# Bias features on three engines, with a second table of logarithms in PSUM, and half of the early weight loads issued later

## The chip, the cores and the metric

The kernel runs on one core of a Trainium2 chip. A core has five engines that work side by side, each through its own list of instructions, in order: TensorE (matrix products, PE in the rows; PEld is its loading of weights), VectorE (DVE), ScalarE (ACT), GpSimd (POOL) and SyncE (SP), which here issues all transfers. Engines meet only through semaphores: an instruction waits until a counter has reached a value, and raises another when it is done. SBUF is the on-chip memory that all of them use; PSUM is the memory that TensorE writes its results to, eight banks of 512 float32 columns on each of 128 partitions, which VectorE and ScalarE also read and write. The metric is device time in microseconds (us) of one execution; lower is better.

## The reference, cut to what matters

Attention with a learned bias on the distance of two positions, followed by two dense layers. What the change touches is the bias:

```python
rel = pos[:, None] - pos[None, :]                  # 576 x 576
psi_rel = log1p(abs(rel))
psi_i = log1p(maximum(pos[:, None], 1.0))
x = (psi_rel / psi_i)[..., None]
h = maximum(x @ w1 + b1, 0.0)                      # 32 hidden units
bias = h @ w2                                      # one number for each of 8 heads
scores = scale * q @ k.T + bias
attn = softmax(scores); out = attn @ v             # 4 sequences, 8 heads, 64 wide
x = (g := x @ w_in) - tanh(g);  x = x @ w_out      # first dense layer
x = (silu(x @ w_gate) * (x @ w_val)) @ w_out2      # second dense layer
```

The bias doesn't depend on the sequence. It is made once, written to memory, and read back for each tile of scores.

## The kernel before, in words

The kernel has three stages. The bias stage takes the first 70 us; then come the attention of the first eight heads without any dense work beside it (to about 130 us), attention and the first dense layer interleaved, and the second dense layer.

**The bias stage.** The logarithm of |row - column| depends on the difference alone, so one table of logarithms (`table`, 1080 columns, each partition with its own shift) holds all rows: a row's logarithms are 576 neighbouring columns of it. Each partition stands for one hidden unit of one of four rows, so that one instruction over 128 x 576 makes 32 hidden units for four rows: a *feature*, max(table x scale, -b1) on VectorE or relu(table x scale + b1) on ScalarE, where scale holds w1 divided by the row's own logarithm. Scale and b1 are operands of one column, [P,1]. VectorE's form lacks the term + b1, which is added as a constant (`fold`) when the result is evacuated.

A *round* is four features, 16 rows. There are 36 rounds (`NQUAD`); six rounds (`GQ`) are one block of 96 rows. In each round:

- VectorE makes features 0 to 2 (`features`, L1073), ScalarE feature 3 (L765), into one of two buffers, `feat[:, par]`, with par the round's parity. Both wait until TensorE has finished round r-2, which read the same buffer (semaphore `e_feat`).
- TensorE (L1345 to L1355) waits for the features and for the evacuation of round r-2, multiplies by w2 in eight matmuls into one of two pairs of PSUM banks, `ps_s` and `ps_y[:, 0:2]`.
- ScalarE evacuates the round before (`evacuate`, L753) into one of six buffers, behind its own feature of this round.
- Every second round SP stores two rounds to memory in four DMAs (`store_bias`, L480); behind rounds 1, 3, 5, 9, 13, 17, 21 and 25 it issues a load of one 512 KB chunk of the first dense layer's weights (`load_w1`, L476). Behind round 27 it issues the first loads of the attention stage (`load_bias`, `load_k`, `load_q`).

The table is made in two parts: the columns that the first six rounds read first, and the rest (0 to `LATE`) during round 0. Rounds from `GQ` on wait for both (`act_tab`, `dve_rest`).

Some small pieces of later work are put into these lists by hand: ScalarE's `q_high` behind its part of rounds 8 and 18 and VectorE's `q_low` (L1082) one round later, ScalarE's `w1_high` in rounds 20 to 23 and VectorE's `w1_low` (L1068) in rounds 21 to 24. `q_low` and `w1_low` read two tensors from SBUF. GpSimd splits two k matrices into a high and a low part at the start (`split_k`, L651) and then has nothing to do until the attention's first `norm` (L671).

**Weights.** The first dense layer's 16 chunks go to a buffer of their own each. Eight are loaded in the bias stage and eight in the interleaved stage, two behind the loads of each head from the tenth on (L587). `w1_high` and `w1_low` split them, 4 tiles in the bias stage and 4 in each interleaved slot, so that one slot uses up two chunks.

**The order** on each engine is written out by hand in these loops; nothing is planned at run time.

Of the kernel before, what the change touches and what calls it, by code (L numbers as in the profile page):

```python
# [27 lines left out]
B, H, S, D = 4, 8, 576, 64  # L28
# [20 lines left out]
GQ = 6  # L49
# [76 lines left out]
def attention_layers_kernel(nc, q_t, k_t, v_p, rowc, w1c, b1c, w2sel, w1_chunks, w2_chunks, out, bias_d, y_d):  # L126
    ctx = ExitStack()
    with ctx:
# [3 lines left out]
        def sem(name):  # L132
            return ctx.enter_context(nc.semaphore(name))
# [20 lines left out]
        with nc.sbuf_tensor("feat", [P, 2, 4, S], F32) as feat:  # L154
# [62 lines left out]
        ps_pt = ctx.enter_context(nc.psum_tensor("ps_pt", [P, 512], F32))  # L217
        ps_s = ctx.enter_context(nc.psum_tensor("ps_s", [P, 2, 512], F32))
        bias_ps = [ps_s, ps_y[:, 0:2, :]]
        gate_ps = [ps_h[:, 0:T2], ps_s[:, 0, 0:T2]]  # L220
        val_ps = [ps_pt[:, 0:T2], ps_s[:, 1, 0:T2]]

# [4 lines left out]
        d_bias = [sem(f"d_bias{i}") for i in range(BR)]  # L227
        d_bias_out, d_y_first, d_y_rest, d_y_in, d_out = [sem(f"d_bias_out{i}") for i in range(EV)], sem("d_y_first"), sem("d_y_rest"), sem("d_y_in"), sem("d_out")
        pool_tab, dve_tab, dve_rest, dve_b, act_tab = (sem(x) for x in ("pool_tab", "dve_tab", "dve_rest", "dve_b", "act_tab"))
        a_feat, v_feat, e_feat, a_bias, e_fold, v_fold = (sem(x) for x in (  # L230
            "a_feat", "v_feat", "e_feat", "a_bias", "e_fold", "v_fold"))
        a_w1hi, v_w1lo, p_w1lo = sem("a_w1hi"), sem("v_w1lo"), sem("p_w1lo")
        a_w2hi, v_w2lo = sem("a_w2hi"), sem("v_w2lo")
        e_score, v_score, a_exp, v_den, v_inv, p_norm = (sem(x) for x in (
# [26 lines left out]
        def bias_groups(rnd):  # L261

            tile, qi = divmod(rnd, GQ)
            return [(tile * ROWSTEP + qi + gg * GQ, TABC - tile * QT - qi - gg * GQ) for gg in range(4)]

        V_FEAT, A_FEAT = (3, 3), (1, 1)

        def feat_done(rnd, per):

            return sum(per[r % 2] for r in range(rnd + 1))  # L270

        def w1_at(k):

# [5 lines left out]

        Q_AT = (8, 18)  # L280
        W1_FIRST, W1_PART, W1_AT = 4, 4, 20
        W1_EARLY, W1_LOAD_AT = 8, (1, 3, 5, 9, 13, 17, 21, 25)
        BIAS_LOADS = 27

        def w1_tiles(moe):
# [184 lines left out]
        def _(eng):  # L470
# [99 lines left out]
            for n in range(H, NH):  # L570
                hd = HEADS[n]
                if hd.unit > 1 and n == FIRST_OF[hd.unit] + 1:
                    store_y(hd.unit - 2, 0)
                load_v(hd)
                following = HEADS[n + 2:n + 3]
                for nxt in following:
                    if not ended(hd):
                        load_q(nxt)
                for t in range(hd.nt):
                    load_bias(hd.tile0 + t + BR)  # L580
                    if t == 1 and hd.unit > 1 and n == FIRST_OF[hd.unit] + 1:
                        store_y(hd.unit - 2, 1)
                for nxt in following:
                    load_k(nxt)
                    if ended(hd):
                        load_q(nxt)
                for c in islice(w1_left, 2 if n > H else 0):  # L587
                    load_w1(c)


# [46 lines left out]
        def _(eng):  # L637
# [84 lines left out]

            split_k(HEADS[0], [])
            split_k(HEADS[1], [])
            eng.wait_ge(e_feat, NQUAD)
            eng.sem_inc(p_glo, CR)
            eng.sem_inc(p_alo, 1)
# [12 lines left out]
        def _(eng):  # L740
# [12 lines left out]
            def evacuate(rnd):  # L753
                par = rnd % 2
                eng.wait_ge(e_feat, rnd + 1)
                if rnd >= 2 * EV and par == 0:
                    eng.wait_ge(d_bias_out[rnd // 2 % EV], 64 * (rnd // 2 // EV))
                eng.activation(pairs(bias_ev[rnd // 2 % EV][:, par, :]), bias_ps[par][:, :, 0:T1], ACT.Identity,
                               bias=fold[:, par:par + 1]).then_inc(a_bias, 1)

            def w1_high(k):
                eng.wait_ge(d_w1[k // 4], 32)
# [2 lines left out]
            def features(rnd):  # L765
                par = rnd % 2
                if rnd >= 2:
                    eng.wait_ge(e_feat, rnd - 1)
                for gg in range(V_FEAT[par], 4):
                    g, col = bias_groups(rnd)[gg]  # L770
                    eng.activation(feat[:, par, gg, :], table[:, col:col + S], ACT.Relu,
                                   scale=scale_t[:, g:g + 1], bias=b1_col).then_inc(a_feat, 1)
# [5 lines left out]
            eng.wait_ge(dve_rest, 2)  # L778
            eng.activation(table[:, 0:LATE], table2[:, 0:LATE], ACT.Ln, bias=1.0).then_inc(act_tab, 1)
            eng.wait_ge(v_fold, 1)  # L780
            for rnd in range(1, NQUAD):
                if rnd == GQ:
                    eng.wait_ge(act_tab, 3)
                    eng.wait_ge(dve_rest, 4)
                features(rnd)
                evacuate(rnd - 1)
                if W1_AT <= rnd < W1_AT + W1_FIRST:
                    w1_high(rnd - W1_AT)
                if rnd in Q_AT:
                    q_high(HEADS[Q_AT.index(rnd)], [])  # L790
# [240 lines left out]
        def _(eng):  # L1031
# [25 lines left out]
            def fold_terms():  # L1057

                eng.tensor_copy(b_cols[:, 0:1], b1_col).then_inc(dve_b, 1)
                eng.tensor_copy(b_cols[:, 1:2], b1_col).then_inc(dve_b, 1)  # L1060
                eng.memset(b_cols[:, 2:4], 0.0).then_inc(dve_b, 1)
                eng.wait_ge(pool_tab, 3)
                distances(slice(0, LATE), dve_rest, 0)
                scales(REST, dve_rest, 2)
                eng.wait_ge(e_fold, 1)
                eng.tensor_copy(fold[:, :], ps_h[:, 0:2]).then_inc(v_fold, 1)
# [6 lines left out]
            def features(rnd):  # L1073
                par = rnd % 2
                if rnd >= 2:
                    eng.wait_ge(e_feat, rnd - 1)
                for gg in range(V_FEAT[par]):
                    g, col = bias_groups(rnd)[gg]
                    eng.tensor_scalar(feat[:, par, gg, :], table[:, col:col + S], scale_t[:, g:g + 1],  # L1079
                                      neg_b1, ALU.mult, ALU.max).then_inc(v_feat, 1)  # L1080

            def q_low(hd, moe):  # L1082
# [7 lines left out]
            eng.wait_ge(dve_tab, 6)  # L1090
            for rnd in range(NQUAD):
                if rnd == GQ:
                    eng.wait_ge(act_tab, 3)
                    eng.wait_ge(dve_rest, 4)
                features(rnd)
                if rnd == 0:
                    fold_terms()
                if W1_AT < rnd <= W1_AT + W1_FIRST:
                    w1_low(rnd - W1_AT - 1)
                if rnd - 1 in Q_AT:  # L1100
                    q_low(HEADS[Q_AT.index(rnd - 1)], [])
# [233 lines left out]
        def _(eng):  # L1335
# [2 lines left out]
            eng.wait_ge(pool_tab, 5)  # L1338

            for gg in range(4):  # L1340
                at = max(0, gg - 1)
                mm = eng.matmul(ps_h[32 * gg:32 * gg + 32, 0:2], sel, b_cols[:, at:at + 2], start=True, stop=True)
            mm.then_inc(e_fold, 1)

            for rnd in range(NQUAD):  # L1345
                par = rnd % 2
                if rnd >= 2:
                    eng.wait_ge(a_bias, rnd - 1)
                eng.wait_ge(v_feat, feat_done(rnd, V_FEAT))
                eng.wait_ge(a_feat, feat_done(rnd, A_FEAT))  # L1350
                for a in range(2):
                    for gg in range(4):
                        mm = eng.matmul(bias_ps[par][32 * gg:32 * gg + 32, a, 0:T1], sel,
                                        feat[:, par, gg, a * T1:(a + 1) * T1], start=True, stop=True)
                mm.then_inc(e_feat, 1)  # L1355
# [283 lines left out]
```

## Time and profile before

| | |
|---|---|
| time, median of 3 runs | 1228.98 us (1228.85 to 1229.46) |
| the profiled execution's own time | 1227.36 us |
| its span, first to last instruction | 1225.5 us |
| busy: TensorE, VectorE, ScalarE, GpSimd | 1176.1, 605.9, 573.2, 525.3 us |
| granted TensorE clock | full speed throughout |
| DMA | 125.46 MB, 102 GB/s on average |

The profile is one execution, recorded by the hardware. An instruction's row gives its start and its duration; the durations of neighbours on an engine overlap a little, so the distance from one start to the next is what an instruction costs in a row of its kind. "[1.46 <-PE ...]" behind a row says how long the engine stood idle ahead of it and which engine ended the wait. The chain of waits starts at the last instruction and goes back, at each step, to what released it. A piece of that chain is work that nothing hid. Rows of one line and kind that follow each other are merged, with their count (x30).

### The profile page before, as it was taken

How to read it: one execution, taken by the hardware profiler on the slowest of the kernel's cores; microseconds unless marked ns; L12 is line 12 of the kernel's file. 1: busy time of each engine (PE TensorE's matmuls, PEld its weight loads, DVE VectorE, ACT ScalarE, POOL GpSimd, SP SyncE). 2: the span in 40 equal slices, each digit the busy share in tenths (PEclk: the TensorE clock that was granted, in tenths of full speed). 3: DMA queues.
4: the chain of work that ended last, by engine and by line, in shares of the span. 5: the costliest groups of instructions: out<-in, count | busy, mean ns of one | idle time of the engine just before them, and what ended most of it. 6: DMA issues, size and time to landing. Idle time of an engine off the chain costs nothing.

```text
span 1225.5 us, 20261 instructions
## 1 busy us (share of the span) xinstructions
PE 1176.1 (96%) x7320; PEld 1079.1 (88%) x7320; DVE 605.9 (49%) x1377; ACT 573.2 (47%) x1163; POOL 525.3 (43%) x584
## 2 busy tenths in 40 slices
PE   5778899999999999999999999999999999999998
PEld 2345699999999998999899999999999999999998
DVE  8967777766665666666666534321211212122111
ACT  6977677665565555555555554422212222121212
POOL 2036577765565557777777622111111111111111
PEclk9999999999999999999999999999999999999999
DMA  5888565353444335455555344200000000000000
GB/s 182 262 253 236 151 197 151 111 146 109 121 134 122 108 89 149 134 140 138 149 140 139 117 143 141 66 26 27 27 1 26 27 26 26 1 26 1 26 1 26
DMA packets 80068, 125.46 MB, mean 102 GB/s; under 512 B 19425, under 2 KB 42977, under 8 KB 79969
## 3 DMA queue, kind: packets, MB, share of 16 engines
q1 hardware_dynamic: 79968, 124.17, 34.4%
q8 instruction: 59, 0.97, 0.3%
q14 instruction: 41, 0.33, 0.1%
HBM read 104.07 MB, written 20.05 MB: 101 GB/s over the span
## 4 chain that ended last, share of the span: by engine, by line
PE 78%; DVE 10%; ACT 4%; issue 4%; SPq 3%; DMA 1%; POOL 0%; DVEq 0%; ACTq 0%; POOLq 0%
PE ps_y L1470 13%; PE ps_s L1565 12%; PE ps_y L1576 12%; PE ps_h L1451 12%; PE ps_h L1565 6%; PE ps_pt L1565 6%; PE ps_pt L1422 5%; PE ps_s L1368 4%; PE ps_pt L1387 4%; DVE feat L1079 3%; DVE prob L1112 2%; PE ps_pt L1451 1%; DVE wbuf L1128 1%; ACT prob L798 1%; DVE g_b L1145 1%
## 5 line engine op out<-in xcount | busy, mean ns | idle before, releaser
L736 POOL TENSOR_TENSOR fr<-tanh_b,fr 128x384 fp32r<-128x384 f32 x72 | 73.1, 1016 | 378.0 <-ACT fr L1009 378.0
L1470 PE MATMUL ps_y<-fr,wbuf 128*128 128x384 f32 x1152 | 226.2, 337 | 0.3 <-POOL fr L681 0.3
L1451 PE MATMUL ps_h<-fr,wbuf 128*128 128x384 f32 x1056 | 205.8, 339 | 0.9 <-DVE fr L1162 0.5
L676 POOL TENSOR_SCALAR prob<-prob,rowinv 128x576 f32<-128x576 f32 (+1 forms) x160 | 126.7, 793 | 184.8 <-DVE rowinv L1123 168.5
L1470 PEld LDWEIGHTS ps_y<-fr,wbuf 128*128 128x128 f32 x1152 | 198.6, 188 | 1.3 <-POOL fr L681 1.2
L1451 PEld LDWEIGHTS ps_h<-fr,wbuf 128*128 128x128 f32 x1056 | 181.0, 188 | 2.0 <-DVE g_b L1145 0.9
L798 ACT ACTIVATE prob<-prob,negmax 128x576 f32<-128x576 f32 (+1 forms) x160 | 124.0, 775 | 116.6 <-DVE negmax L1112 116.1
L1576 PE MATMUL ps_y<-wbuf,fr 128*128 128x512 f32 x648 | 161.1, 393 | 0.0
L681 POOL TENSOR_TENSOR fr<-g_b,fr 128x384 fp32r<-128x384 f32 x96 | 100.5, 1047 | 115.7 <-ACT fr L829 115.7
L1576 PEld LDWEIGHTS ps_y<-wbuf,fr 128*128 128x128 f32 x648 | 120.6, 188 | 22.1
L1128 DVE TENSOR_TENSOR wbuf<-ps_pt,wbuf 128x512 fp32r<-128x512 f32 (+1 forms) x136 | 91.5, 673 | 46.9 <-ACT wbuf L812 45.2
L1112 DVE CUSTOM_DVE_ANT_0 prob<-ps_s,biasb 128x576 f32<-128x576 f32 (+1 forms) x147 | 110.0, 748 | 7.5 <-PE ps_s L1368 3.7
L1313 DVE TENSOR_TENSOR g_b<-ps_h,g_b 128x384 f32<-128x384 f32 x36 | 20.0, 556 | 180.3 <-ACT g_b L1006 180.3
L1313 DVE TENSOR_TENSOR g_b<-ps_s,g_b 128x384 f32<-128x384 f32 x36 | 20.0, 556 | 159.7 <-ACT g_b L1006 159.7
L1387 PE MATMUL ps_pt<-ident,prob 128*128 128x128 f32 (+1 forms) x640 | 86.6, 262 | 5.3 <-DVE xy_stage L1153 2.4
L812 ACT ACTIVATE wbuf<-ps_pt 128x512 fp32r<-128x512 f32 (+1 forms) x136 | 78.5, 577 | 26.5 <-PE ps_pt L1387 25.4
L660 POOL TENSOR_TENSOR fr<-raw,wbuf 128x576 fp32r<-128x576 f32 x59 | 87.0, 1475 | 4.9
L1387 PEld LDWEIGHTS ps_pt<-ident,prob 128*128 128x128 f32 (+1 forms) x640 | 68.8, 140 | 20.2 <-issue 13.3
L1006 ACT ACTIVATE g_b<-ps_h 128x384 f32<-128x384 f32 x36 | 17.7, 492 | 140.5 <-PE ps_pt L1565 140.5
L1422 PE MATMUL ps_pt<-wbuf,fr 128*128 128x192 f32 (+1 forms) x512 | 80.8, 302 | 0.5 <-DVE wbuf L1128 0.3
L1009 ACT ACTIVATE fr<-tanh_b 128x384 fp32r<-128x384 f32 x72 | 37.9, 526 | 89.4 <-DVE tanh_b L1316 87.7
L1565 PE MATMUL ps_s<-fr,wbuf 128*128 128x384 f32 x432 | 78.2, 335 | 0.0
(134 smaller groups left out, 1940.8 us busy)
## 6 DMA issues: line engine op xcount, KB each, us to landing
biasb<-bias_scratch SPq DMA_DIRECT2D x128, 216.0 KB, 2.8
raw<-k_t SPq DMA_DIRECT2D x59, 288.0 KB, 3.1
bias_scratch<-w_raw SPq DMA_DIRECT2D x72, 144.0 KB, 3.2
biasb<-bias_scratch SPq DMA_DIRECT2D x64, 144.0 KB, 2.9
w_raw<-w_chunks SPq DMA_DIRECT2D x16, 512.0 KB, 5.7
prob<-w_chunks SPq DMA_DIRECT2D x8, 768.0 KB, 4.4
raw<-v_p SPq DMA_DIRECT2D x32, 160.0 KB, 2.3
biasb<-bias_scratch SPq DMA_DIRECT2D x64, 72.0 KB, 2.7
```

What stands on the lines that cost most here:

```text
L660: eng.tensor_tensor(lo, src, hi.bitcast(F32), ALU.subtract).then_inc(p_klo, 1)
L676: eng.tensor_scalar(row, row, rowinv[0:hd.rows, tile % PR:tile % PR + 1], 1.0, ALU.mult, ALU.mult).then_inc(p_norm, 1)
L681: eng.tensor_tensor(g_lo[c % 2], g_b[:, c % 2, :], g_hi[c % 2].bitcast(F32), ALU.subtract)\
L798: eng.activation(row, row, ACT.Exp, scale=-1.0, bias=negmax[0:hd.rows, col], accum_out=rowsum[0:hd.rows, col]).then_inc(a_exp, 1)
L1112: eng.tensor_tensor_reduce(out=pairs(prob[rows, i, :]), in0=score_bank(tile, moe)[rows, :, 0:T1], in1=pairs(biasb[rows, tile % BR, :]), sc ...
L1128: eng.tensor_tensor(lo, by_chunk(pt_bank(t, moe), hd), hi.bitcast(F32), ALU.subtract).then_inc(v_pt, 1)
L1387: mm = eng.transpose(bank[:, c * hd.rows:(c + 1) * hd.rows], prob[rows, tile % PR, KEY0[c]:KEY0[c] + P], ident[rows, rows])
L1422: mm = eng.matmul(bank, vv[:, c, :, :].rearrange("p a d -> p (a d)"), pt_of(hd, part)[:, c, :], start=part == 0 and c == 0, stop=not ended ...
L1451: mm = eng.matmul(hidden_bank(u, c)[:, 0:TOK], w[:, cols], x[:, d, :], start=d == 0 and i == 0, stop=d == KC - 1 and i == 2)
L1470: mm = eng.matmul(ps_y[:, d, 0:TOK], w[:, cols], g[c % 2], start=c == 0 and i == 0, stop=c == C1 - 1 and i == 2)
L1565: mm = eng.matmul(bank, w[:, cols], y[:, d, :], start=d == 0 and i == 0, stop=d == KC - 1 and i == 2)
L1576: mm = eng.matmul(ps_y[:, t, :], a[c % 2][:, t * P:(t + 1) * P], w, start=c == 0 and i == 0, stop=c == C2 - 1 and i == 2)
```

## The change

1. A second table, `table_ps`, lies in the two PSUM banks `ps_y[:, 2:4]`, which the bias stage did not use: ScalarE computes it with two Ln instructions of 512 columns behind its evacuation of round 0. From round 6 on VectorE's features read it in place of `table`; ScalarE's and GpSimd's read `table`.
2. From round 6 on the four features of a round are split by `feature_split`, as (VectorE, GpSimd, ScalarE): (2, 1, 1), (2, 2, 0) and (1, 2, 1) in rounds whose number leaves 0, 1 and 2 when divided by 3. Of twelve features VectorE makes five, GpSimd five and ScalarE two; it was nine, none and three. Rounds 0 to 5 keep (3, 0, 1). TensorE also waits for GpSimd's features (`p_feat`). The constant that ScalarE adds follows the number of its own features.
3. `W1_EARLY` goes from 8 to 4: chunks 0 to 3 are loaded behind rounds 1, 3, 11 and 19, and chunks 4 to 15 two at a time behind the loads of each head from the ninth on.

```diff
+        table_ps = ps_y[:, 2:4, :].rearrange("p b n -> p (b n)")
...
-        V_FEAT, A_FEAT = (3, 3), (1, 1)
-
-        def feat_done(rnd, per):
-
-            return sum(per[r % 2] for r in range(rnd + 1))
+        def feature_split(rnd):
+
+            return (3, 0, 1) if rnd < GQ else ((2, 1, 1), (2, 2, 0), (1, 2, 1))[rnd % 3]
+
+        def feat_done(rnd, engine):
+
+            return sum(feature_split(r)[engine] for r in range(rnd + 1))
...
-        W1_EARLY, W1_LOAD_AT = 8, (1, 3, 5, 9, 13, 17, 21, 25)
+        W1_EARLY, W1_LOAD_AT = 4, (1, 3, 11, 19)
...
-                for c in islice(w1_left, 2 if n > H else 0):
+                for c in islice(w1_left, 2):
                     load_w1(c)
...                                                          # GpSimd
             split_k(HEADS[1], [])
+            eng.wait_ge(act_tab, 3)
+            eng.wait_ge(dve_rest, 4)
+            for rnd in range(GQ, NQUAD):
+                eng.wait_ge(e_feat, rnd - 1)
+                of_vector, own, _ = feature_split(rnd)
+                for gg in range(of_vector, of_vector + own):
+                    g, col = bias_groups(rnd)[gg]
+                    eng.tensor_scalar(feat[:, rnd % 2, gg, :], table[:, col:col + S], scale_t[:, g:g + 1],
+                                      neg_b1, ALU.mult, ALU.max).then_inc(p_feat, 1)
...                                                          # ScalarE
-                               bias=fold[:, par:par + 1]).then_inc(a_bias, 1)
+                               bias=fold[:, feature_split(rnd)[2]:feature_split(rnd)[2] + 1]).then_inc(a_bias, 1)
...
-                for gg in range(V_FEAT[par], 4):
+                for gg in range(4 - feature_split(rnd)[2], 4):
...
-            for rnd in range(1, NQUAD):
+            features(1)
+            evacuate(0)
+            for half in (slice(0, 512), slice(512, 1024)):
+                eng.activation(table_ps[:, half], table2[:, half], ACT.Ln, bias=1.0).then_inc(act_tab, 1)
+            for rnd in range(2, NQUAD):
...                                                          # VectorE
-                for gg in range(V_FEAT[par]):
+                source = table if rnd < GQ else table_ps
+                for gg in range(feature_split(rnd)[0]):
                     g, col = bias_groups(rnd)[gg]
-                    eng.tensor_scalar(feat[:, par, gg, :], table[:, col:col + S], scale_t[:, g:g + 1],
+                    eng.tensor_scalar(feat[:, par, gg, :], source[:, col:col + S], scale_t[:, g:g + 1],
                                       neg_b1, ALU.mult, ALU.max).then_inc(v_feat, 1)
...
-                    eng.wait_ge(act_tab, 3)
+                    eng.wait_ge(act_tab, 5)
...                                                          # TensorE
-                at = max(0, gg - 1)
+                at = 1 if gg == 3 else 0
...
-                eng.wait_ge(v_feat, feat_done(rnd, V_FEAT))
-                eng.wait_ge(a_feat, feat_done(rnd, A_FEAT))
+                eng.wait_ge(v_feat, feat_done(rnd, 0))
+                if rnd >= GQ:
+                    eng.wait_ge(p_feat, feat_done(rnd, 1))
+                eng.wait_ge(a_feat, feat_done(rnd, 2))
```

## Rows read from the trace of the kernel before

**Rows 1.** The chain of waits in order of time: start us, us, what.
```profile
26.38 14.79 DVE feat L1079 x30
41.21 0.56 DVE wbuf L1086
...
44.83 0.60 DVE wbuf L1071
```

**Rows 2.** Busy time by engine in one stretch, then clock, DMA share, GB/s.
```profile
20.00:40.00 20.00, 15.78 (x212) 8.12 (x215) 19.93 (x41) 19.61 (x28) 0.00 (x0) 1.00 0.90 291
```

**Rows 3.** Groups by shape, 0 to 115 us: count, busy us, mean ns, idle before.
```profile
L1079 DVE TENSOR_SCALAR feat<-prob 128x576 f32<-128x576 f32 x108 | 54.1, 578 | 1.0 <-PE ps_y L1353 0.8
L771 ACT ACTIVATE feat<-prob,raw 128x576 f32<-128x576 f32 x36 | 30.9, 857 | 1.3 <-DVE prob L1066 0.8 <-DVE prob L1055 0.5
...
L676 POOL TENSOR_SCALAR prob<-prob,rowinv 128x576 f32<-128x576 f32 x19 | 14.0, 746 | 76.1 <-DVE rowinv L1123 76.1
...
L758 ACT ACTIVATE w_raw<-ps_s,prob 128x576 f32<-128x576 f32 x18 | 13.3, 737 | 0.8 <-PE ps_s L1353 0.7
...
L1133 DVE COPY w_raw<-ps_h 64x384 f32<-64x384 f32 x5 | 2.8, 560 | 0.2
...
L1038 DVE TENSOR_SCALAR prob<-prob,raw 128x600 f32<-128x600 f32 x1 | 0.5, 524 | 0.0
...
L1034 DVE TENSOR_SCALAR prob<-prob,raw 128x144 f32<-128x144 f32 x1 | 0.3, 294 | 2.8 <-POOL ident L647 2.8
...
L1066 DVE COPY prob<-ps_h 128x2 f32<-128x2 f32 x1 | 0.1, 146 | 0.0
```

**Rows 4.** Timeline of the bias stage: start us, us, engine, line, [idle before].
```profile
13.06 2.15 PE L1353 MATMUL ps_y<-feat,prob 128*32 128x288 f32 x16 [3.01 <-DVE feat L1079]
...
15.29 0.74 ACT L758 ACTIVATE w_raw<-ps_y,prob 128x576 f32<-128x576 f32 x1 [1.46 <-PE ps_y L1353]
...
28.04 1.21 PE L1353 MATMUL ps_s<-feat,prob 128*32 128x288 f32 x16 [0.59 <-DVE feat L1079]
...
29.31 0.74 ACT L758 ACTIVATE w_raw<-ps_s,prob 128x576 f32<-128x576 f32 x1 [0.30 <-PE ps_s L1353]
```

**Rows 5.** Timeline of the first attention slots, GpSimd and VectorE.
```profile
75.25 0.16 DVE L1123 RECIPROCAL rowinv<-rowsum 128x1 f32<-128x1 f32 x1
...
75.62 0.74 POOL L676 TENSOR_SCALAR prob<-prob,rowinv 128x576 f32<-128x576 f32 x1 [1.33 <-DVE rowinv L1123]
...
77.09 1.41 POOL L660 TENSOR_TENSOR wbuf<-w_raw,wbuf 128x576 fp32r<-128x576 f32 x1
...
77.60 1.32 DVE L1086 SCALAR_TENSOR_TENSOR wbuf<-w_raw,wbuf 64x384 fp32r<-64x384 f32 x1
...
79.50 1.46 POOL L676 TENSOR_SCALAR prob<-prob,rowinv 128x576 f32<-128x576 f32 x2 [1.00 <-DVE rowinv L1123]
...
80.37 0.56 DVE L1133 COPY w_raw<-ps_h 64x384 f32<-64x384 f32 x1
...
83.81 0.67 POOL L658 TENSOR_SCALAR wbuf<-raw 128x576 fp32r<-128x576 f32 x1 [1.24 <-DMA raw<-k_t]
```

**Rows 6.** Timeline of SP's queue: start us, us, line, what is issued, count.
```profile
58.19 1.95 SPq L486 DMA_DIRECT2D bias_scratch<-w_raw  x4
...
72.43 3.02 SPq L486 DMA_DIRECT2D bias_scratch<-w_raw  x4
...
137.87 0.43 SPq L506 DMA_DIRECT2D raw<-q_t  x1
...
142.31 0.33 SPq L525 DMA_DIRECT2D raw<-v_p  x1
```

**Rows 7.** DMA issues of the page: count, KB each, us to landing.
```profile
w_raw<-w_chunks SPq DMA_DIRECT2D x16, 512.0 KB, 5.7
```

**Rows 8.** Timeline of ScalarE in the second interleaved slot.
```profile
157.91 0.62 ACT L763 ACTIVATE wbuf<-w_raw 128x512 fp32r<-128x512 f32 x1
```

More of the change, by code:

```diff
@@ L229, in attention_layers_kernel @@
         pool_tab, dve_tab, dve_rest, dve_b, act_tab = (sem(x) for x in ("pool_tab", "dve_tab", "dve_rest", "dve_b", "act_tab"))
-        a_feat, v_feat, e_feat, a_bias, e_fold, v_fold = (sem(x) for x in (
-            "a_feat", "v_feat", "e_feat", "a_bias", "e_fold", "v_fold"))
+        a_feat, v_feat, p_feat, e_feat, a_bias, e_fold, v_fold = (sem(x) for x in (
+            "a_feat", "v_feat", "p_feat", "e_feat", "a_bias", "e_fold", "v_fold"))
         a_w1hi, v_w1lo, p_w1lo = sem("a_w1hi"), sem("v_w1lo"), sem("p_w1lo")
@@ L1060, in fold_terms @@
                 eng.tensor_copy(b_cols[:, 1:2], b1_col).then_inc(dve_b, 1)
-                eng.memset(b_cols[:, 2:4], 0.0).then_inc(dve_b, 1)
+                eng.memset(b_cols[:, 2:3], 0.0).then_inc(dve_b, 1)
                 eng.wait_ge(pool_tab, 3)
```

## The prediction

> **What bounds the kernel now.** I read the page first (engine shares, the 40 slices, the chain by line), then the chain of waits in order of time, then the busy time of each engine in the bias stage, then the groups by shape and the timeline of single rounds. TensorE is 96% busy over the span, but not in the first 70 us, and the change touches only those and some loads. In the chain the bias stage is one run of VectorE features: 30 of them in 14.79 us, 0.493 us each, broken only by VectorE's own extra pieces, 0.56 us for a q_low and 0.60 us for a w1_low [rows 1]. In a stretch of 20 us VectorE is busy 19.93, ScalarE 19.61, GpSimd 0 and TensorE 15.78 [rows 2]. So a round costs three features, 3 x 0.493 = 1.478 us; ScalarE is as full, and GpSimd is free. That invites moving work to GpSimd.
>
> A second limit lies right under the first and is in no share of busy time. A feature buffer is used again two rounds later, so features(r) waits for TensorE's round r-2. TensorE needs 1.21 us for a round; from VectorE's last issue to TensorE's start lie 0.085 us (a feature is recorded at 0.578 us and the next starts after 0.493) [rows 1, 3] and about 0.10; the engine that waits for TensorE starts 0.06 us (28.04 + 1.21 to 29.31) to 0.08 us (13.06 + 2.15 to 15.29) after its end [rows 4]. The ring over two rounds is 1.478 + 0.185 + 1.21 + 0.08 = 2.95, 1.477 a round: the same as VectorE's load. A better balance helps only if this ring gets shorter too.
>
> **The change, part by part.** *One feature from PSUM.* Half-rate reading shows in the two shapes with one [P,1] operand: 600 columns take 0.524 us and 144 take 0.294, 0.504 ns a column [rows 3]. Copies from PSUM take 0.560 us for 384 columns and 0.146 for 2, 1.08 ns a column [rows 3]. Twice 0.504 is 1.01, so a full-rate column is 1.01 to 1.08 ns; with 1.04 the 576 columns cost 0.30 us more: 0.493 + 0.30 = 0.79 us a feature. Bounds: w1_low's 0.60 for 512 columns [rows 1] makes 0.60 + 64 x 1.04 = 0.67 if the two [P,1] operands cost nothing behind a PSUM read; 0.578 + 0.30 = 0.88 if nothing overlaps. I take 0.79, since it changes only the column rate of the very instruction that is moved.
>
> The Trainium skill (VectorE: DVE Perf Modes, "Why PSUM operands drop a tier") says that a float32 operand in PSUM leaves only the one-column rate; the copies above agree. The sum needs only the rows.
>
> *One feature on GpSimd.* A tensor_scalar of 576 columns takes 0.67 us with two immediates [rows 5] and 0.746 with one [P,1] operand [rows 3]; with two I estimate 0.80, bounds 0.74 and 0.88. It starts 0.21 us after its releaser (75.25 + 0.16 to 75.62) [rows 5].
>
> *The new ring.* From round 6 the split of three rounds is (2,1,1), (2,2,0), (1,2,1). VectorE does four features in a row in the first two, but can't begin the next four until TensorE has done the second of these rounds. That makes three rounds cost 4 x 0.79 + 0.185 + 1.21 + 0.08 = 4.64 us. GpSimd has its own four in a row (second and third round): 4 x 0.80 + 0.21 + 0.06 + 1.21 = 4.68, with 0.06 for its hand-over to TensorE as an estimate from ScalarE's. Both are longer than their loads (5 x 0.79 = 3.95 and 5 x 0.80 = 4.00), and longer than before, 3 x 1.478 = 4.43. I take 4.65: +0.22 for each of ten such groups (rounds 6 to 35), **+2.2 us**. ScalarE, 2 x 0.857 + 3 x 0.737 = 3.93 at most [rows 3], no longer bounds; TensorE's 3.63 doesn't either.
>
> *VectorE's extra pieces.* Before, two q_low and four w1_low lay whole on the path: 2 x 0.56 + 4 x 0.60 = 3.52. Now VectorE idles 4.65 - 3.95 = 0.70 us in each group, ahead of its run of four. The pieces behind rounds 9, 21 and 24 fall inside a run and still cost 0.56 + 0.60 + 0.60; the one behind round 19 fits the idle time; those behind 22 and 23 share one gap and stick out by 1.20 - 0.70 = 0.50. Sum 2.26: **-1.26 us**.
>
> *What these pieces meet.* They read two SBUF tensors, and GpSimd now runs beside them. The q_low at 77.60 took 1.32 us instead of 0.56: GpSimd's instruction ran from 77.09 to 78.50, and VectorE's ended 0.42 after it [rows 5]. A copy from PSUM at 80.37 inside GpSimd's pair (79.50, 1.46 us) kept its 0.56 [rows 5], so I charge the features nothing. For a piece the bounds are 0 and 0.76. GpSimd is there 4.0/4.65 = 86% of the time; half of 0.80 is left on average, 0.34, less the 0.1 or so of a start that isn't held: 0.25. On the path that is three times 0.25, twice 0.25 in the shared gap, and 0.56 + 0.25 - 0.70 = 0.11 behind round 19: **+1.3 us**.
>
> *The second table.* Two Ln of 512 columns, each about as long as a ScalarE pass over as many (under 0.74, which 576 take [rows 3]), go behind evacuate(0), where ScalarE then stood idle 1.46 us [rows 4]; at most 0.1 us sticks out. Without that gap they would cost 1.2 to 1.5 us once. VectorE first needs the table five rounds later. The fold columns cost nothing.
>
> *The weights that load later.* Four early loads of 512 KB leave a stage whose DMA engines are 90% busy [rows 2]; nothing on the path waits for those loads there. The next two chunks are now issued behind the q loads at 137.87, where SP's next row in this view is a v load at 142.31 [rows 6]; two issues fit between. Landing takes 5.7 us [rows 7], so about 145, and ScalarE first takes them at 157.91 [rows 8]: 12 us of cover. Cost 0; were the cover gone, the stage would slip by what is missing.
>
> *What the delay does later.* At round 27 seven groups are done, 1.5 - 1.26 + 1.3 = +1.6; at round 35 it is 2.2 - 1.26 + 1.3 = +2.2. SP issues round 27's store when it is evacuated (58.19) [rows 6], so its stream of loads for the attention slots starts 1.6 late; the first score, which waits for round 35, comes 2.2 late. Behind both, the attention slots run at SP's pace and the layers at TensorE's; I see nothing that gives it back. Between the two ends, with the tables: **+1.9 us**. The profiled execution took 1227.36 us (span 1225.5), so 1229.3 for one like it; the median of the runs shown is 1.62 higher, so 1230.9.
>
> **Rivals.** *A, the ring is short (faster).* With features at 0.67 VectorE's ring is 4 x 0.67 + 1.475 = 4.15, and GpSimd's with 0.74 and a hand-over of 0.06 is 4 x 0.74 + 0.06 + 0.06 + 1.21 = 4.29: ten groups save 1.4. VectorE then idles 4.29 - 3.35 = 0.94 a group and isn't the bound, so most of the 3.52 goes: about 2.0 after holds. 1228.98 - 3.4 = 1225.6; with GpSimd at 0.80 only 1227.5. For it: the 0.60 of w1_low. Against: both low ends are needed at once, and GpSimd's [P,1] operand does show its price.
>
> *B, GpSimd holds VectorE (slower).* Place: the six pieces with two SBUF inputs. Price: 0.76 each instead of 0.25 adds 5 x 0.51 + 0.5 = 3.1, so 1230.9 + 3.1 = 1234.0. It decides from a mean hold of about 0.37: five on the path then add 0.6 to the forecast's 1.9. For it: 77.60. Against: that was a GpSimd instruction of 1.41 us, and these are of 0.80.
>
> *C, the PSUM read has a larger fixed part (slower).* At 0.86 a feature the group is 4 x 0.86 + 1.475 = 4.92, +4.9 for ten; the idle time shrinks to 0.62 (0.2 more on the path): 1230.9 + 2.9 = 1233.8. Against it: the copy of 2 columns from PSUM takes only 0.146 [rows 3]. The Trainium skill (Perfetto Trace Analysis, "Optimizing Scalar/DVE Operations") gives VectorE some 125 ns of access overhead a PSUM instruction and 60 an SBUF one; by that a feature would be 0.79 + 0.065, this case. The row of 2 columns speaks against it.
>
> *D, the lighter queue pays back.* SP's store of four DMAs takes 3.02 at 72.43 and 1.95 at 58.19 [rows 6]. If fewer weights in flight remove that 1.1, the sum is 1229.8. Against: the last early load was issued ahead of 58.19, and lands in 5.7 [rows 7].
>
> **How the numbers follow.** A measurement of this kernel can't tell less than about 0.2%, 2.46 us, from no change: 1226.5 to 1231.4. The forecast has 0.55; its own range, 1229.0 to 1232.5 (features 0.76 to 0.82, holds 0.1 to 0.35), crosses the upper edge, so I put 0.40 of it inside and 0.15 above. A 0.17, all faster; B 0.12 and C 0.09, slower; D 0.07, same. Faster 0.17, same 0.40 + 0.07 = 0.47, slower 0.36. The range, 1226.2 to 1233.9, reaches halfway into A and nearly to B and C.
>
> **What would show it.** Right: features at about 0.88 us recorded and 0.79 apart, VectorE idle some 0.7 us every three rounds until TensorE's round ends, groups of three rounds at 4.65 us, rounds 9, 21 and 24 longer, w1_low at 0.9 us, SP's store of round 27 at about 59.8 and the first score 2 us later. Wrong: a group below 4.43 us, GpSimd or VectorE without gaps from round 6 on (then load and not the ring bounds), features stretched while GpSimd runs, or a plain attention stage whose length changes by more than 1 us.

## The result, and the profile after

The changed kernel takes 1297.7 us (median of 5 runs, 1296.82 to 1298.02) against 1228.98 before: ratio 1.0556, 95% interval 1.0544 to 1.0568. The forecast was 1230.9, with a range that ended at 1233.9. The profiled execution took 1297.93 us, its span 1295.9.

The time sits in one place. In the bias stage a GpSimd feature takes 2.29 us, where I had estimated 0.80; a VectorE feature from PSUM takes what was forecast. Both groups of features, by line (duration of one in ns, minimum/median/maximum):

```profile
L735 POOL TENSOR_SCALAR feat<-prob x50: 2279/2287/2380, 20.8 to 134.5; 128x576 f32<-128x576 f32 x50
```

```profile
L1096 DVE TENSOR_SCALAR feat<-ps_y,prob x50: 866/876/879, 20.7 to 129.8; 128x576 f32<-128x576 f32 x50
```

The chain of waits after, in order of time (start us, us, what), answers to [rows 1]:

```profile
34.71 9.10 POOL feat L735 x4
43.81 0.25 issue
44.06 2.19 PE ps_y L1372 x16
46.24 0.09 issue
46.34 9.10 POOL feat L735 x4
```

This is the ring that the forecast drew for GpSimd, with another size in it: four features in a row, the hand-over, TensorE's round, the next four. From 34.71 to 46.34 it lasts 11.63 us: 9.10 + 0.25 + 2.19 + 0.09. The forecast's was 4.68. But GpSimd hardly waits in it. Its timeline has five features in a row, behind an idle time of 0.27 us:

```profile
46.34 11.35 POOL L735 TENSOR_SCALAR feat<-prob 128x576 f32<-128x576 f32 x5 [0.27 <-PE ps_y L1372]
```

So its load alone, five features at 2.275 us from start to start, is 11.37 of the 11.63 us. The waits of the ring add 0.26.

TensorE's round has also become longer, 2.15 us instead of 1.21. The timeline of TensorE where that begins (start us, us, line, tiles; the last bracket is the idle time before it and what ended it):

```profile
20.84 1.21 PE L1372 MATMUL ps_y<-feat,prob 128*32 128x288 f32 x16 [0.26 <-DVE feat L1096]
23.36 1.21 PE L1372 MATMUL ps_s<-feat,prob 128*32 128x288 f32 x16 [1.32 <-DVE feat L1096]
27.91 2.16 PE L1372 MATMUL ps_y<-feat,prob 128*32 128x288 f32 x16 [3.33 <-POOL feat L735]
32.43 2.15 PE L1372 MATMUL ps_s<-feat,prob 128*32 128x288 f32 x16 [2.37 <-POOL feat L735]
```

And the busy times by stretch (PE, PEld, DVE, ACT, POOL, then granted clock, DMA share, GB/s), the first of which answers to [rows 2]:

```profile
20.00:40.00 20.00, 9.93 (x97) 3.66 (x93) 9.60 (x13) 8.48 (x12) 19.00 (x9) 0.68 0.53 157
28.00:44.00 16.00, 8.53 (x64) 2.65 (x64) 6.42 (x8) 5.64 (x8) 15.82 (x8) 0.50 0.30 77
40.00:60.00 20.00, 11.99 (x96) 3.90 (x88) 7.52 (x9) 5.97 (x8) 19.46 (x9) 0.59 0.36 101
...
160.00:180.00 20.00, 16.46 (x108) 11.35 (x107) 14.24 (x45) 14.59 (x33) 12.68 (x15) 1.00 0.82 231
```

GpSimd went from 0 to 19 us of 20, VectorE from 19.93 to 9.60 and ScalarE from 19.61 to 8.48. The full engines of before now wait for the free one. The granted clock has a mean of 0.59 from 40 to 60 us; between 28 and 44 us it is 0.50, the 1.2 GHz level. It is at the 2.4 GHz level again by 160 us, once the stage is over. It fell between the rounds at 23.36 and 27.91, where TensorE was idle for 3.33 us after an idle time of 1.32. From 17.90 us until then rounds took 1.21 us. The length of a round alone doesn't tell the level, though: the round at 14.02 took 2.16 us, and the one at 13.06 before took 2.15 [rows 4], where the profile gives a granted clock of 1.00.

The sum closes within 2 us: ten groups at 11.62 instead of 4.43 are +71.9; VectorE's extra pieces, 3.52 us on the path before, are now wholly beside GpSimd, which makes +68.4. The first score starts at 139.10 instead of 69.05, 70.05 us later, and the span is 70.4 longer. So what the stage lost was passed on one to one. Of the 1.7 us by which 70.1 exceeds the sum, 0.95 lie ahead of round 6, which VectorE began at 20.74 us here and at 19.79 in the trace of the kernel before. They aren't the change's: in the run below with the later loads alone, whose features are those of the kernel before, round 6 began at 20.92. The other 0.7 I don't place.

### The profile page after: what moved, and what is told of

It is laid out like the page before. It is cut to its first block, busy times and chain, and to the rows that moved or that the text cites. A ratio compares the mean times of both kernels' runs of the same rounds, so it can differ in the third digit from the quotient of the medians.

```text
span 1295.9 us, 20300 instructions
## 1 busy us (share of the span) xinstructions
PE 1202.4 (93%) x7320; PEld 1082.4 (84%) x7320; DVE 602.5 (46%) x1337; ACT 568.1 (44%) x1155; POOL 639.8 (49%) x634
## 4 chain that ended last, share of the span: by engine, by line
PE 76%; POOL 8%; DVE 7%; issue 3%; ACT 3%; SPq 2%; DMA 1%; DVEq 0%; ACTq 0%; POOLq 0%
PE ps_y L1489 12%; PE ps_s L1584 12%; PE ps_y L1595 12%; PE ps_h L1470 11%; POOL feat L735 7%; PE ps_h L1584 6%; PE ps_pt L1584 6%; PE ps_pt L1441 5%; PE ps_s L1387 4%; PE ps_pt L1406 4%; DVE prob L1129 2%; PE ps_pt L1470 1%; DVE wbuf L1145 1%; ACT prob L814 1%; PE ps_y L1372 1%
## 5 line engine op out<-in xcount | busy, mean ns | idle before, releaser
L735 POOL TENSOR_SCALAR feat<-prob 128x576 f32<-128x576 f32 x50 | 113.7, 2291 | 12.3 <-PE ps_s L1372 11.3
L1584 PE MATMUL ps_s<-y_odd,wbuf 128*128 128x384 f32 x432 | 78.2, 335 | 0.0
```

Of the source, the lines that this page charges most:

```text
L735: eng.tensor_scalar(feat[:, rnd % 2, gg, :], table[:, col:col + S], scale_t[:, g:g + 1], neg_b1, ALU.mult, ALU.max).then_inc(p_feat, 1)
L1584: mm = eng.matmul(bank, w[:, cols], y[:, d, :], start=d == 0 and i == 0, stop=d == KC - 1 and i == 2)
```

## The experiments

Was it the form of GpSimd's instruction, its two [P,1] operands, the odd start of its columns, or other engines' traffic? Nine forms, run by GpSimd on the same table into unused memory, beside a VectorE that makes three features a round from PSUM:

```diff
-return (3, 0, 1) if rnd < GQ else ((2, 1, 1), (2, 2, 0), (1, 2, 1))[rnd % 3]
+return (3, 0, 1)
...
+for _ in range(3):
+    eng.tensor_scalar(next(at), odd, one, neg_b1, ALU.mult, ALU.max).then_inc(p_try, 1)
+for _ in range(3):
+    eng.tensor_scalar(next(at), even, one, neg_b1, ALU.mult, ALU.max).then_inc(p_try, 1)
...
```

> The table in PSUM stays, but VectorE makes three features of every round and ScalarE one, as before; GpSimd makes none and instead runs nine forms of tensor_scalar over 576 columns into unused memory, three times each, so that each form is timed by itself. In the changed kernel a GpSimd feature (mult by a [P,1] column, then max with a [P,1] column, first column odd) took 2.29 us and a known form (mult, mult, one [P,1]) 0.75. Theory F (the pair mult, max): the four forms with max after mult take 2.3 us whatever their operands, the mult,mult and mult,add forms 0.67 to 0.81. Theory P (the second [P,1] operand): the forms with two columns take 2.3, those with one or none 0.75, max or not. Theory A (the odd first column): only the form that begins at column 384 is fast. Theory C (VectorE or TensorE beside it): all forms are slow, or slow where VectorE runs. For the whole: VectorE's three PSUM features cost 3 x 0.79 = 2.37 us a round against 1.48, for 30 rounds +26.8 us, so about 1256 us, more if TensorE's clock falls.

The forms come in this order, three times each: mult,max with two columns from an odd start; the same from column 384; mult,max with one column; mult,max with immediates; mult,mult and mult,add with two columns; (left out: mult,mult with one column, 2.19); max alone; mult,mult with immediates. Timeline of GpSimd (the duration is that of all three):

```profile
24.99 6.85 POOL L742 TENSOR_SCALAR w_raw<-prob 128x576 f32<-128x576 f32 x3 [14.24 <-PE ps_s L1394]
31.82 6.83 POOL L744 TENSOR_SCALAR w_raw<-prob 128x576 f32<-128x576 f32 x3
38.62 6.58 POOL L746 TENSOR_SCALAR w_raw<-prob 128x576 f32<-128x576 f32 x3
45.17 6.34 POOL L748 TENSOR_SCALAR w_raw<-prob 128x576 f32<-128x576 f32 x3
51.50 2.44 POOL L750 TENSOR_SCALAR w_raw<-prob 128x576 f32<-128x576 f32 x3
53.91 2.44 POOL L752 TENSOR_SCALAR w_raw<-prob 128x576 f32<-128x576 f32 x3
...
58.49 4.89 POOL L756 TENSOR_SCALAR w_raw<-prob 128x576 f32<-128x576 f32 x3
63.34 1.95 POOL L758 TENSOR_SCALAR w_raw<-prob 128x576 f32<-128x576 f32 x3
```

The start column changes nothing (6.85 and 6.83). A [P,1] operand costs 0.08 us each (2.44, 2.19, 1.95 over three). Replacing max by mult or add takes two thirds away: 2.28 us becomes 0.81, as theory F had it. Contention as the cause of 2.28 is out, since neighbours of the same stretch differ by that much. The one execution took 1260.44 us (about 1256 expected, more if the clock falls): three PSUM features a round fill VectorE, 20.00 of 20 us. It also tells of the clock: in this stretch GpSimd works only 5.30 of 20 us, and the granted clock has the same mean as in the changed kernel:

```profile
60.00:80.00 20.00, 12.47 (x101) 4.38 (x105) 20.00 (x26) 9.54 (x14) 5.30 (x6) 0.59 0.37 101
```

Is max alone the whole loss? The changed kernel with one word replaced:

```diff
-neg_b1, ALU.mult, ALU.max).then_inc(p_feat, 1)
+neg_b1, ALU.mult, ALU.add).then_inc(p_feat, 1)
```

> The changed kernel with one word exchanged: add in place of max in GpSimd's features, with the same two [P,1] columns, the same table columns and waits (GpSimd's five of twelve features lack the relu). If the maximum alone made the loss: GpSimd's features 0.81 us, groups of three rounds 4.6 to 4.7 us, TensorE's clock nearly full, 1230.5 to 1231.5 us against 1297.7. If the place or the operands made it: 1290 or more.

It takes 1230.81 us, ratio 1.0010 (1.0001 to 1.0020) to the kernel before: all but 2 of the 69 us are gone. The duration of its GpSimd features, and its chain:

```profile
L735 POOL TENSOR_SCALAR feat<-prob x50: 817/827/1403, 20.9 to 70.7; 128x576 f32<-128x576 f32 x50
```

```profile
53.80 3.25 POOL feat L735 x4
57.05 0.25 issue
57.30 1.24 PE ps_s L1372 x16
58.54 0.09 issue
58.63 3.26 POOL feat L735 x4
```

The group is 4.83 us here, where 4.6 to 4.7 was expected, and GpSimd's ring is the longer one. The other fast form, mult,mult with the second operand an immediate, shows VectorE's:

```diff
-neg_b1, ALU.mult, ALU.max).then_inc(p_feat, 1)
+1.0, ALU.mult, ALU.mult).then_inc(p_feat, 1)
```

> The changed kernel with one operand of GpSimd's features exchanged: mult by the [P,1] column, then mult by 1.0 in place of max with -b1, so GpSimd's five of twelve features lack the relu. This form took 0.75 us elsewhere in the trace. If the size of GpSimd's feature is the whole error, everything else of the forecast holds: groups of three rounds at 4.64 us (VectorE's four features of 0.79 in a row, then TensorE's round), TensorE's clock at full speed, time 1230 to 1231 us. If GpSimd's features are slow for another reason (contention, the wait between engines), they stay near 2.3 us and the time near 1298. If loads and not the ring bound, groups take 4.0 us and the time is about 1224.

1230.67 us, ratio 1.0011 (1.0002 to 1.0020). The trace is of the longest of the eleven executions, 1233.62 us. GpSimd's feature has a median of 0.745 us, and the chain runs through VectorE:

```profile
31.52 3.24 DVE feat L1096 x4
34.76 0.09 issue
34.85 1.24 PE ps_y L1372 x16
36.12 3.25 DVE feat L1096 x4
```

A group is 4.60 us, where the forecast had 4.64 for this ring. With either fast form the total is within 0.3 us of the forecast's 1230.9.

The later loads alone, on the kernel before:

```diff
-W1_EARLY, W1_LOAD_AT = 8, (1, 3, 5, 9, 13, 17, 21, 25)
+W1_EARLY, W1_LOAD_AT = 4, (1, 3, 11, 19)
...
-for c in islice(w1_left, 2 if n > H else 0):
+for c in islice(w1_left, 2):
```

> Only the third part of the change, in the kernel before: chunks 0 to 3 of the weights load behind rounds 1, 3, 11, 19, the other twelve two at a time from the ninth head on. My account: nothing waits for these loads at either place, 1229.0 us within 1 us. Rival D (the lighter queue pays back): SP's slow store of 3.0 us at 72 falls to about 2 and the time to 1227.9 or less. If the later loads were in the way: w1_high in the second interleaved slot would wait, and the time would rise by what is missing.

1228.87 us, ratio 0.9999 (0.9989 to 1.0008): no loss and no gain beyond that interval, which is about 1 us to either side. That alone doesn't exclude rival D's 1.1 us, but SP's slow store does: it takes 3.01 us here and took 3.02 [rows 6].

```profile
73.47 3.01 SPq L486 DMA_DIRECT2D bias_scratch<-w_raw  x4
```

Is the ring, and not the load, what keeps the fast form from a gain? A third feature buffer lets round r start once round r-3 is done (edit on the mult,mult kernel, shown for VectorE; the other engines alike):

```diff
+third = w1_raw[2][:, :, :, :, :].rearrange("p c i s n -> p (c i s n)")[:, 0:4 * S]...
+def feat_of(rnd):
+    return third if rnd % 3 == 2 else feat[:, rnd % 3, :, :]
...
-if rnd >= 2:
-    eng.wait_ge(e_feat, rnd - 1)
+if rnd >= 3:
+    eng.wait_ge(e_feat, rnd - 2)
```

> The kernel with mult, mult by 1.0 on GpSimd (its features lack the relu; 1230.67 us) with a third buffer of features, so that features(r) wait for TensorE's round r-3. My ring: with two buffers a group of three rounds took VectorE's four features in a row, 3.24, and TensorE's round, 1.24 and hand-overs, 4.60 us; with three it falls to VectorE's load of 5 x 0.79 = 3.95 to 4.0 us, and the extra pieces lie fully on the path again: round 35 ends some 2.9 us earlier, about 1227.8 us. Rival: TensorE's round or ScalarE bounds it and the time stays within 0.5 us of 1230.7.

1228.05 us, ratio 0.9993 (0.9984 to 1.0003), 2.6 below the same form with two buffers; the two intervals just touch. Between VectorE's features there is no idle time left in this stretch; five start every 3.92 us (28.25, 32.17), 5 x 0.79 as forecast for the load:

```profile
28.25 0.87 DVE L1102 TENSOR_SCALAR w_raw<-ps_y,prob 128x576 f32<-128x576 f32 x1
...
32.17 0.87 DVE L1102 TENSOR_SCALAR w_raw<-ps_y,prob 128x576 f32<-128x576 f32 x1
```

But the stage doesn't run at that pace. From 22 to 40 us the chain passes ScalarE's features and evacuations and TensorE's rounds, in turn (L789 makes features, into w_raw where that is the third buffer; L776 evacuates):

```profile
26.94 1.24 PE ps_y L1378 x16
28.27 0.74 ACT w_raw L776
29.01 0.75 ACT w_raw L789
29.76 0.68 ACT w_raw L776
30.44 0.76 ACT feat L789
31.34 1.24 PE ps_s L1378 x16
```

That is 4.40 us for three rounds, a ring through ScalarE that was hidden under the 4.60; from there to 70 us VectorE is in the chain only around its pieces (41 to 51 us). So the expected time, 1227.8, came out without the expected group of 3.95 to 4.0, which is in part luck. Even with a fast form and a third buffer the kernel only comes level with the one before.

What is the table in PSUM worth? The mult,mult kernel with VectorE reading the SBUF table:

```diff
-source = table if rnd < GQ else table_ps
+source = table
```

> The kernel with mult, mult by 1.0 on GpSimd (its features lack the relu; 1230.67 us), but VectorE reads the table in SBUF throughout, as in the kernel before; the table in PSUM is still made. If VectorE's half-rate read and GpSimd exclude each other: the two share one time, 5 x 0.49 + 5 x 0.75 = 6.2 us for three rounds or, where they overlap in part, 5 to 6, so 1234 to 1246 us, and features of 0.58 us are recorded at up to 1.3. If they don't: VectorE's ring is 4 x 0.49 + 1.475 = 3.4 and GpSimd's 4 x 0.77 + 1.4 = 4.5, about 1229 us.

1233.1 us, ratio 1.0034 (1.0022 to 1.0046), 2.4 above the same with the PSUM table. That lies between the two times expected, 1229 without mutual holds and 1234 to 1246 with them. VectorE's features now last 0.907 us in the median of all 68 (18 of them from the rounds before GpSimd joins in) instead of 0.575 without a neighbour, and GpSimd's 0.942 instead of 0.745. Two engines on the SBUF table hold each other, and reading PSUM at 0.79 a feature is the cheaper of the two.

Is there a fast form that takes a maximum? Six more forms in the frame of the nine:

```diff
+eng.tensor_scalar(next(at), odd, one, neg_b1, ALU.mult, ALU.min).then_inc(p_try, 1)
...
+eng.tensor_scalar(next(at), odd, one, None, ALU.mult).then_inc(p_try, 1)
...
+eng.tensor_relu(next(at), odd).then_inc(p_try, 1)
...
```

> As the first run of forms (VectorE makes three features a round from PSUM, GpSimd none), with six other forms on GpSimd, 576 columns, three times each: mult then min with two [P,1] columns; mult alone with a column; mult then is_gt; the product of two tensors; a relu instruction; a maximum with 0 on the same bits read as int32. Measured so far: mult,max 2.28 us, mult,mult and mult,add 0.81, max alone 1.63. Theory S (whatever compares or selects is slow on GpSimd): min 2.3, is_gt and relu over 1.5, int32 max over 1.5, mult alone under 0.75. Theory M (only the float maximum is): min, is_gt, relu or the int32 maximum come under 0.9, and with the fastest of them a relu on GpSimd would be affordable.

GpSimd's timeline: mult,min with two columns; mult alone; (left out: mult,is_gt, 6.84); a product of two tensors; relu; (left out: an int32 max, 4.88).

```profile
24.88 6.83 POOL L742 TENSOR_SCALAR w_raw<-prob 128x576 f32<-128x576 f32 x3 [14.04 <-PE ps_s L1388]
31.69 5.14 POOL L744 TENSOR_SCALAR w_raw<-prob 128x576 f32<-128x576 f32 x3
...
43.61 3.53 POOL L748 TENSOR_TENSOR w_raw<-prob 128x576 f32<-128x576 f32 x3
47.10 4.89 POOL L750 TENSOR_SCALAR w_raw<-prob 128x576 f32<-128x576 f32 x3
```

None is fast: min and is_gt cost what max costs, relu 1.63 us. The second row upsets theory S, which had it under 0.75: a mult alone takes 1.71 us, twice a mult followed by another mult. So it isn't that a maximum is dear and the rest cheap. The one execution took 1255.81 us.

The last run separates "a maximum is slow" from "only a pair of mult and add is fast", and looks at VectorE's SBUF reads beside both:

```diff
+eng.tensor_scalar(next(at), odd, 0.5, None, ALU.mult).then_inc(p_try, 1)
...
+eng.tensor_scalar(next(at), odd, 0.5, 0.5, ALU.mult, ALU.add).then_inc(p_try, 1)
...
+eng.tensor_scalar(next(at), odd, 0.0, 0.5, ALU.max, ALU.mult).then_inc(p_try, 1)
...
-source = table if rnd < GQ else table_ps
+source = table
```

> As the run of nine forms, but VectorE makes its three features a round from the SBUF table, as the kernel before does, so that what GpSimd's forms do to VectorE's SBUF reads is seen too. GpSimd runs, on 576 columns of the table into scratch: mult,max with two columns (4 times), mult,mult with two columns (6), and with immediates mult alone, add alone, mult,add, add,mult, max,mult and max,max (3 each). Theory M (a maximum or comparison makes GpSimd slow): mult alone and add alone take at most 0.65 us like mult,mult; max,mult and max,max 2.1. Theory P (only a pair of mult and add is fast, every other form is slow): mult alone and add alone take 1.63 like max alone, mult,add and add,mult 0.65, max,mult and max,max 2.1. On VectorE: if GpSimd holds it whatever the form, its SBUF features, 0.578 recorded in the kernel before, take 0.7 to 0.8 beside every form; if only the fast forms take the shared read, they stay near 0.58 beside the 9 us of mult,max and reach 0.7 to 0.8 beside mult,mult. The stage should end near that of the kernel before unless VectorE is held; the scratch work takes no part in the result.

GpSimd's timeline: mult,max (x4) and mult,mult (x6) with two columns; with immediates mult alone, (left out: add alone, 6.14), mult,add, (left out: add,mult, 2.54), max,mult, (left out: max,max, 7.75):

```profile
24.30 11.04 POOL L742 TENSOR_SCALAR w_raw<-prob 128x576 f32<-128x576 f32 x4 [13.54 <-PE ps_s L1392]
35.32 6.03 POOL L744 TENSOR_SCALAR w_raw<-prob 128x576 f32<-128x576 f32 x6
41.32 6.47 POOL L746 TENSOR_SCALAR w_raw<-prob 128x576 f32<-128x576 f32 x3
...
53.87 2.54 POOL L750 TENSOR_SCALAR w_raw<-prob 128x576 f32<-128x576 f32 x3
...
58.89 7.79 POOL L754 TENSOR_SCALAR w_raw<-prob 128x576 f32<-128x576 f32 x3
```

Theory P holds for the forms tried: only pairs of mult and add are fast (beside a VectorE that reads SBUF, 0.85 us with immediates and 1.00 with two columns); one operation alone takes 2.05 to 2.16, and anything with a maximum 2.58 to 2.76. VectorE in the same run, in four stretches:

```profile
28.97 4.21 DVE L1116 TENSOR_SCALAR feat<-prob 128x576 f32<-128x576 f32 x6
...
34.61 7.05 DVE L1116 TENSOR_SCALAR feat<-prob 128x576 f32<-128x576 f32 x7
...
43.98 8.42 DVE L1116 TENSOR_SCALAR feat<-prob 128x576 f32<-128x576 f32 x12 [0.17 <-PE ps_s L1392]
...
53.36 5.04 DVE L1116 TENSOR_SCALAR feat<-prob 128x576 f32<-128x576 f32 x6
```

Features come 0.69 us apart beside mult,max (4.21 less the 0.085 by which a record outlasts the next start, over 6), 1.00 beside mult,mult with two columns, 0.69 beside the single operations and 0.83 beside the fast pairs with immediates, instead of 0.493 [rows 1]. The slow forms hold VectorE too, though less. The one execution took 1244.68 us.

That leaves no version of this change that I expect to beat the kernel before, and I ran none. One maximum on GpSimd beside SBUF features costs 2.76 us of GpSimd; in it VectorE makes four features, each 0.20 later, and loses 0.8 us for a feature that would have cost it 0.493. From PSUM, VectorE's eight others of twelve would take 8 x 0.79 = 6.3 us against a group of 4.43. This is argued from rows, not run.

## Why the prediction was wrong

The step that failed is "One feature on GpSimd". It took 0.67 us for two immediates and 0.746 for one [P,1] operand and went on to 0.80 for two. That slope is right: 0.65, 0.73, 0.81 for mult,mult in the run of nine forms. But both rows were of instructions whose two operations are mult,mult (lines 658 and 676), and the moved one is mult,max. The rows differed from the feature in the operation as well as in the operands, and I carried over only the operands. So the bounds, 0.74 to 0.88, were bounds on the wrong thing: no row before shows a maximum on GpSimd at all. A much slower kind of row of that engine and shape was there and should have been the upper bound, an instruction of 576 columns with two tensor inputs at 1.41 us [rows 5]. With it GpSimd's ring is 4 x 1.41 + 1.48 = 7.1 us, and ten groups less the hidden pieces make 26.9 - 3.5 = +23 us. Even that bound lies below the 2.29, but it would have given the rival that was missing: GpSimd itself becomes the bound by a wide margin.

What the runs showed in place of 0.80 is 2.29 us a feature. With it, one sentence of "The new ring" falls too: that both rings are longer than their loads. GpSimd's load, put at 4.00 us a group, became 11.37, and the ring around it 11.63.

The other steps, read from the runs in which GpSimd is fast:

- *One feature from PSUM*: 0.79 us apart (3.24 for four, less what the last overlaps), as forecast. Rival C, 0.86, is refuted. The Trainium skill (Perfetto Trace Analysis, "Optimizing Scalar/DVE Operations") gives VectorE about 125 ns of overhead on PSUM and 60 on SBUF; the 0.065 us more a feature that would follow isn't there.
- *The new ring*: VectorE's 4.60 (forecast 4.64). GpSimd's 4.83 with a feature of 0.81 (forecast 4.68 with 0.80); GpSimd's hand-over to TensorE takes 0.25 us, not the 0.06 that I took from ScalarE, and it starts 0.09 us after TensorE, not 0.21. The same 0.25 and 0.09 stand in the chain of the changed kernel.
- *The load, and the extra pieces*: with a third buffer VectorE makes five features in 3.92 us, so with two buffers the ring and not this load was the bound, as the step said; VectorE idled 0.58 (mult,mult) and 0.77 us (mult,add) a group, where I had 0.70. What the step lacks is the ring through ScalarE, 4.40, which bounds next. Rival A wanted a ring of 4.29 from faster features; VectorE's weren't faster, and even with a third buffer the time is 1228.05, not its 1225.6.
- *Holds of two-input pieces*: in the mult,mult run the q_low pieces took 0.98 and 0.98 instead of 0.56, and the four w1_low 0.68, 1.02, 1.16 and 0.85 instead of 0.68: 0.31 more on average, where I had 0.25. In the mult,add run one q_low took 1.08 and no other piece was held. The size differs from piece to piece and run to run; rival B, 0.76 each, is refuted.
- *The second table*: in the changed kernel two Ln in 1.10 us at 13.93; one feature later ScalarE still idles 0.42 until TensorE's round ends. It costs nothing that shows, as forecast.
- *The weights that load later*: nothing, as forecast. Rival D is refuted by the store that stays at 3.01 us.
- *What the delay does later*: one to one over 70 us: from the first score to the end lie 1156.5 us before and 1156.8 after. For 2 us the traces can't tell, since that stretch lasts 1155.7 us in the mult,add run and 1158.0 in the mult,mult run.
- Not in the forecast at all: TensorE's clock. Its round grew from 1.24 to 2.19 us in the chain, 0.95 of the 7.0 us by which the ring exceeds the forecast; 5.9 are the four features and 0.1 the hand-overs. It cost little of the time, though. With a round of 1.24 the ring would be 10.68 us, less than GpSimd's load of 11.37, so the longer round made a group longer by 0.26 us at most. This is argued from rows, not run.

With a GpSimd feature of 0.75 to 0.81 us instead of 2.29 the forecast's time comes out: 1230.67 and 1230.81 measured, 1230.9 forecast. So the size of that one term is what failed. That the two times lie within 0.3 us of the forecast is in part luck. Both intervals are 0.2% wide, more than the whole +1.9 us that was forecast. And in the traces, counted from the start of round 6, the first score comes 2.9 us later than before in the mult,add run and 3.4 in the mult,mult run, where the forecast had 2.2.

## What to carry to other kernels

A duration may be carried from one instruction to another only if engine, shape, operands *and operations* agree; where the operation has no row, that price is the unknown of the forecast, and the range has to reach at least to the slowest row of that engine and shape. Before work is moved to an idle engine, run the very instruction there once, in scratch, beside the kernel: that alone would have decided this change. And ask of each engine what it becomes if its price is wrong by three: here the idle engine's load, 4.00 us a group in the forecast, became 11.37 and the bound of the stage.

## What the runs showed of the hardware

- On GpSimd, with VectorE reading PSUM beside it, 576 float32 columns take 0.65 us for a pair of mult and add with immediates, but 1.63 for a maximum or a relu alone, 1.71 for a mult alone with one [P,1] operand, and 2.11 for mult,max with immediates. An instruction that does less (mult alone) is more than twice as long as a pair (1.71 against 0.73 to 0.81). Why, no run here shows. The Trainium skill (GPSIMD Engine Reference, 4.1 Engine selection) names add, mult and maximum in one breath and calls operations with one input roughly line-rate. These rows differ: with immediates the forms lie a factor of 2.5 (maximum alone) to 3.2 (mult,max) above the pair.
- A GpSimd feature that waits for TensorE starts 0.09 us after it, and TensorE starts 0.25 us after GpSimd's end.
- VectorE instructions with one SBUF input are slowed while GpSimd runs: they come 0.69 to 1.00 us apart instead of 0.493, and GpSimd's own mult,max goes from 2.28 to 2.76. The Trainium skill (SBUF — State Buffer, "Who interferes with whom") says that when VectorE uses both of its ports, whoever issues first has the shared pair of ports for its whole instruction and blocks the other. Beside mult,mult with two columns that would fit: there both engines take 1.00 us an instruction. Beside 2.76 us instructions VectorE still ended a feature every 0.69 us, so it can't be the case here for the whole of such an instruction.
- In the changed kernel's bias stage, where TensorE waits 2 to 3 us between many of its rounds, the granted clock was 0.50 (the 1.2 GHz level) between 28 and 44 us, and a round took 2.15 us instead of 1.21. In the run of nine forms, where TensorE waits for VectorE and ScalarE, mostly 1.15 us or less, it was 0.59 between 60 and 80 us; in the run of six forms, with mostly the same waits of 1.15 us, it was 1.00 between 20 and 40 us. So the waits alone don't tell the level, and why it differs no run here shows.
